# A joint between two runs: weight sums moved to GpSimd, T2's low part by halves, P1 and P6 ahead of the first groups

## The reference

```python
# attention with decay: per head, blocks of 64 tokens, a state carried over
intra = (qb @ kb.T * Dmask) @ vb
inter = (qb * lam_pow) @ kv_state
# mixture: 4 experts, w1[e] 512x1024, w2[e] 1024x512
out += p[:, e:e + 1] * (np.maximum(x @ w1[e], 0.0) @ w2[e])
# projection: two factors, then two matrices
h = (x @ w1) * (x @ w2) @ w3
return h @ w_out
```

## Time and profile before

| what | value |
|---|---|
| median of 3 runs | 796.5 us (796.08 to 797.36) |
| the profiled execution's own time | 793.99 us |
| its span (first to last instruction) | 792.2 us |
| TensorE busy | 776.9 us, 98% |
| VectorE, GpSimd, ScalarE busy | 442.4, 439.7, 207.8 us |
| granted TensorE clock | 1.000 |

### The profile page before, as it was taken

How to read it: one execution, slowest core, us unless ns; L and a number is a source line. 1 busy time by engine, 2 the same in 40 slices (tenths; PEclk the granted TensorE clock), 3 DMA queues, 4 the chain that set the end, 5 groups by cost and what they waited for, 6 DMA issues and landing times.

```text
span 792.2 us, 9983 instructions
## 1 busy us (share of the span) xinstructions
PE 776.9 (98%) x3854; PEld 642.5 (81%) x3854; DVE 442.4 (56%) x627; ACT 207.8 (26%) x292; POOL 439.7 (56%) x389
## 2 busy tenths in 40 slices
PE   9999889999999999999999999999998899999998
PEld 7878768888888888888888888888886788888887
DVE  7549874554545545545545455456378653636356
ACT  7423331122222212221222122122234331223110
POOL 8837586557546565665575565656657533342500
PEclk9999999999999999999999999999999999999999
DMA  9977111010210110210100111101000200100004
GB/s 336 342 260 235 61 73 53 2 53 27 67 53 1 54 55 0 86 40 22 53 23 32 53 41 54 54 0 54 27 26 1 72 11 25 54 28 0 1 1 159
DMA packets 26590, 51.29 MB, mean 65 GB/s; under 512 B 3112, under 2 KB 9008, under 8 KB 26544
## 3 DMA queue, kind: packets, MB, share of 16 engines
q1 hardware_dynamic: 26384, 50.64, 18.9%
q10 hardware_dynamic: 160, 0.02, 0.0%
HBM read 45.38 MB, written 5.28 MB: 64 GB/s over the span
## 4 chain that ended last, share of the span: by engine, by line
PE 92%; DVE 4%; POOL 2%; issue 1%; ACT 0%; ACTq 0%; DVEq 0%
PE banks L1303 41%; PE banks L1276 27%; PE banks L1286 15%; PE banks L1189 5%; PE banks L1201 1%; DVE probs L869 1%; PE banks L1233 1%; PE banks L1225 1%; DVE qs L879 1%; POOL xs_l L524 1%; POOL hl L524 1%; PE banks L1249 0%; DVE t L908 0%; PE banks L1241 0%; POOL w_l L524 0%
## 5 line engine op out<-in xcount | busy, mean ns | idle before, releaser
L1010 DVE TENSOR_TENSOR acc<-banks,acc 128x512 f32<-128x512 f32 x215 | 147.1, 690 | 148.3 <-PE banks L1303 135.8
L524 POOL TENSOR_TENSOR hl<-ring,hh 128x512 fp32r<-128x512 f32 x96 | 138.3, 1454 | 162.1 <-ACT hh L630 162.1
L630 ACT ACTIVATE hh<-ring 128x512 fp32r<-128x512 f32 x120 | 75.7, 632 | 404.6 <-DVE ring L987 345.8
L524 POOL TENSOR_TENSOR w_l<-up_raw,w_h 128x1024 fp32r<-128x1024 f32 x43 | 103.4, 2406 | 90.8 <-ACT w_h L630 90.8
L1303 PE MATMUL banks<-hh,d_h 128*128 128x512 f32 x384 | 149.5, 389 | 2.0 <-POOL hl L524 2.0
L1303 PE MATMUL banks<-hh,d_l 128*128 128x512 f32 x384 | 149.4, 389 | 0.0
L1303 PE MATMUL banks<-hl,d_h 128*128 128x512 f32 x384 | 149.4, 389 | 0.0
L1276 PE MATMUL banks<-xs_h,w_h 128*128 128x512 f32 x336 | 131.2, 390 | 5.5 <-DVE u L968 4.7
L1276 PE MATMUL banks<-xs_h,w_l 128*128 128x512 f32 x336 | 130.8, 389 | 0.0
L1276 PE MATMUL banks<-xs_l,w_h 128*128 128x512 f32 x336 | 130.7, 389 | 0.0
L1303 PEld LDWEIGHTS banks<-hh,d_h 128*128 128x128 f32 x384 | 72.1, 188 | 17.3 <-issue 2.4
(11 more groups left out here) (139 smaller groups left out, 992.7 us busy)
## 6 DMA issues: line engine op xcount, KB each, us to landing
dn_raw<-in_moe_w SPq DMA_DIRECT2D x16, 512.0 KB, 3.3
up_raw<-in_moe_w SPq DMA_DIRECT2D x14, 512.0 KB, 3.3
w_raw<-in_w3T SPq DMA_DIRECT2D x16, 256.0 KB, 6.4
up_raw<-in_w SPq DMA_DIRECT2D x8, 512.0 KB, 3.3
pb<-route_scratch SPq DMA_DIRECT2D x12, 256.0 KB, 3.3
out<-acc SPq DMA_DIRECT2D x11, 256.0 KB, 2.0
wo_raw<-in_w_out SPq DMA_DIRECT2D x8, 256.0 KB, 5.3
chunk_w<-in_kT SPq DMA_DIRECT2D x8, 256.0 KB, 5.3
```

The lines of the kernel that those rows point to most:

```text
L524: return tt(dst, whole, high.bitcast(F32), ALU.subtract)
L630: return nc.scalar.activation(dst, src, ACT.Copy)
L1010: tt(cols, group_bank(g), cols, ALU.add).then_inc(acc_done, 1)
```

## The change

Three things.

At the start, GpSimd makes only the first half of T2's low part; VectorE makes the second half behind `t3_sum(0)`, with a semaphore of its own, `t2_lo`, and the counts of `tp_lo` fall by one. 

For w = 1, TensorE does P1 and P6 first and then groups 0 to 3; VectorE's `sum_u2(1)` goes ahead of the adds of these groups, and GpSimd does `d_low(0)` behind `hidden_low` 2 and not behind `hidden_low` 1.

At the joint, the four sums of run 17's weights go from VectorE to GpSimd, behind `a_low(17)` and ahead of B11's low parts; ScalarE's `s_high(17)` goes from behind the copy of P2 to between the `b_high` of B11 and of B21; VectorE's `weight_sums_low(17)` goes from behind `sum_c22(16)` to between `t4_sum(1)` and `t3_low(1)`.

```diff
--- before.py
+++ after.py
@@ -254,7 +254,8 @@
 
 
         b_hi, b_lo, xc_hi, xc_lo = sem("b_hi"), sem("b_lo"), sem("xc_hi"), sem("xc_lo")
-        t_sum, t_hi, tp_lo, t3_lo = sem("t_sum"), sem("t_hi"), sem("tp_lo"), sem("t3_lo")
+        t_sum, t_hi, tp_lo, t2_lo, t3_lo = (
+            sem("t_sum"), sem("t_hi"), sem("tp_lo"), sem("t2_lo"), sem("t3_lo"))
 
 
         wa_hi, wa_lo, ws_sum, ws_hi, ws_lo = sem("wa_hi"), sem("wa_lo"), sem("ws_sum"), sem("ws_hi"), sem("ws_lo")
@@ -559,7 +560,9 @@
                     low(xs_l[:, which, k, :], src[:, k, :], xs_h[:, which, k, :]).then_inc(tp_lo, 1)
 
             T2_AT, T4_AT = acc[:, 0:KH, 0:CW], acc[:, KH:KT, 0:CW]
-            t_low(0, T2, T2_AT)
+
+            pool.wait_ge(t_hi, 2)
+            low(xs_l[:, T2, 0, :], T2_AT[:, 0, :], xs_h[:, T2, 0, :]).then_inc(tp_lo, 1)
             t_low(0, T4, T4_AT)
 
             def a_low(j):
@@ -601,12 +604,17 @@
                 if later:
                     s_low(w + 1)
                 hidden_low(OUTS * w + 1)
-                d_low(w)
-                for k in range(2, OUTS):
+                if w > 0:
+                    d_low(w)
+                hidden_low(OUTS * w + 2)
+                if w == 0:
+                    d_low(w)
+                for k in range(3, OUTS):
                     hidden_low(OUTS * w + k)
 
 
             a_low(NQ + 1)
+            sums(NQ + 1)
             for which, rows in ((B11, slice(0, KH)), (B21, slice(KH, KT))):
                 for k in range(KH):
                     pool.wait_ge(b_hi, NB + 1 + (which == B21))
@@ -762,6 +770,7 @@
             for d in range(KT):
                 xc_high(d)
             b_high(B11, slice(0, KH), slice(0, CW), grouped(NQ - 1, 0) - KH)
+            s_high(NQ + 1)
             b_high(B21, slice(KH, KT), slice(0, CW), grouped(NQ - 1, 0))
             t_high(1, 0)
 
@@ -784,7 +793,6 @@
                         t_high(1, 3)
                         factor(5, "Ub", bank_u)
                         factor(0, "P2", bank_x)
-                        s_high(w + 1)
                         d_high(hidden_of(w))
                     else:
                         snapshot(w)
@@ -953,6 +961,8 @@
             third_low(NCH - 1)
             t2_sum(0)
             t3_sum(0)
+            dve.wait_ge(t_hi, 2)
+            sub(xs_l[:, T2, 1, :], acc[:, 1, 0:CW], xs_h[:, T2, 1, :]).then_inc(t2_lo, 1)
 
             def sum_u2(w):
                 dve.wait_ge(piece_done, made(w, "P6"))
@@ -1001,9 +1011,10 @@
                 cols = acc[:, d, c * CW:(c + 1) * CW] if Q < NQ else outs[:, ST * c + d, :]
                 if g == 0:
 
-                    dve.wait_ge(tp_lo, 6)
+                    dve.wait_ge(tp_lo, 5)
+                    dve.wait_ge(t2_lo, 1)
                 if g == GR * NQ:
-                    dve.wait_ge(tp_lo, 12)
+                    dve.wait_ge(tp_lo, 11)
                 if Q in (0, NQ):
                     nc.vector.tensor_copy(cols, group_bank(g)).then_inc(acc_done, 1)
                 else:
@@ -1052,8 +1063,11 @@
                     sum_u2(w)
                     gate_piece(2, "Ub", bank_u)
                 else:
-                    add_groups(w - 1, (0, 1, 2, 3))
+                    if w > 1:
+                        add_groups(w - 1, (0, 1, 2, 3))
                     sum_u2(w)
+                    if w == 1:
+                        add_groups(w - 1, (0, 1, 2, 3))
                     add_groups(w - 1, (4, 5))
                     gate_piece(0, "Ua", bank_u)
                     add_groups(w - 1, (6, 7))
@@ -1081,6 +1095,7 @@
             t2_sum(1)
             t3_sum(1)
             t4_sum(1)
+            weight_sums_low(NQ + 1)
             t3_low(1)
 
             def b22_low():
@@ -1103,14 +1118,11 @@
                     sum_u2(w)
                     if w == NQ:
                         b22_low()
-                        weight_sums(w + 1)
                     add_groups(before, (4, 5, 6, 7))
                     sum_u3(w)
 
                     dve.wait_ge(h_lo, n)
                     sum_c22(w, a_tile[3])
-                    if w == NQ:
-                        weight_sums_low(w + 1)
                     sum_c21(w, a_tile[1])
                     sum_c12(w, a_tile[2])
                 else:
@@ -1341,7 +1353,9 @@
                     pe.wait_ge(probs_ready, 2 * NCH)
                 pe.wait_ge(ws_lo, w + 1)
                 if w in (0, NQ):
-                    pe.wait_ge(tp_lo, 4 if w == 0 else 8)
+                    pe.wait_ge(tp_lo, 3 if w == 0 else 7)
+                if w == 0:
+                    pe.wait_ge(t2_lo, 1)
                 product(bank_y, w % 2, S2, T2, True)
 
             def ua(w):
@@ -1380,14 +1394,14 @@
                 else:
                     pe.wait_ge(xc_lo, ST)
                 if w == NQ:
-                    pe.wait_ge(tp_lo, 10)
+                    pe.wait_ge(tp_lo, 9)
                 product(bank_z, w % 2, S1, T1, True)
 
             def p4(w):
 
                 pe.wait_ge(u3_ready, w + 1)
                 if w in (0, NQ):
-                    pe.wait_ge(tp_lo, 6 if w == 0 else 12)
+                    pe.wait_ge(tp_lo, 5 if w == 0 else 11)
                 product(bank_y, w % 2, A22, T4, False)
 
             def p3(w):
@@ -1409,10 +1423,16 @@
             p3(0)
 
             for w in range(1, NQ):
-                groups(w - 1, (0, 1))
-                p1(w)
-                groups(w - 1, (2, 3))
-                p6(w)
+                if w == 1:
+
+                    p1(w)
+                    p6(w)
+                    groups(w - 1, (0, 1, 2, 3))
+                else:
+                    groups(w - 1, (0, 1))
+                    p1(w)
+                    groups(w - 1, (2, 3))
+                    p6(w)
                 groups(w - 1, (4, 5))
                 ua(w)
                 groups(w - 1, (6, 7))
```

## The result

The kernel after takes 791.37 us (median of 4 runs, 791.08 to 791.79) against 796.93 us (4 runs, 796.08 to 798.42): ratio 0.9929, interval 0.9911 to 0.9946. The profiled executions tell another story: span 792.2 before, 789.3 after, 2.9 us apart, as forecast (789.35). So the steps of the sum have to be read first, and then the question is why the medians are 2.7 us further apart than the traces.

The account below looks back on a forecast made before the run. TensorE, busy 98% of the span, was taken as the bound, so only its waits could be gained. Start 2.45 plus joint 0.4 made 2.85 us, taken from the 796.5 median: 793.6, range 791.3 to 795.9.

Parts of the forecast that it names:

- The start: First run, up to the first groups: T2 by halves and P1(1), P6(1) ahead gain 2.45 us, bounds 1.2 and 2.8.
- GpSimd's set: Start: T4 x2, `hl` x2, `d_l` and one more `hl`, needed by the first groups; to end between 112.2 and 113.3.
- up to 0.15 more: Start, P6(0): added to its 0.50 wait because the pipe no longer drains; 0.6 taken.
- this is why moving `d_low` matters: Start: with `d_low` behind `hl` 2 the multiply ends by 109.9, `c21` by 110.6, so P6(1) doesn't wait.
- The joint: Runs 16 and 17: P4(16) at 614.2 instead of 614.60, 0.4 us gained of 3.13; bounds 3.2 gain, 1.0 loss.
- over a microsecond: Joint: P6(16) waits this long for `xs_l` in place of 0.34, at no net cost.
- the slide of B21 onto `t1_sum`: Joint: B21's two subtractions slide from 596 onto `t1_sum` and `t2_sum`, putting VectorE's sums up to 1.2 us later.
- `t4_sum` under T2's first subtraction: Joint: `t4_sum`, made later by B21, falls inside GpSimd's chain and costs up to 1.0 us more.
- bounds of 613.7 - 603.07 = 10.6 and 11.7: Joint: GpSimd's six subtractions from 603.07 with three VectorE operations end at 613.7; `t4_sum` inside adds up to 1.0.
- The sum: Whole kernel: 2.45 + 0.4 = 2.85 us off the profiled execution, span 792.2 to 789.35.
- Rival B: Joint freed: P4(16) starts when P5 is done, 3.2 us gained instead of 0.4, 790.85; chance 0.13.
- its last step: Whole kernel: the profiled execution is 2.5 us below the 796.5 median, from which the same 2.85 is taken: 793.6.

## Why the prediction was wrong, point by point

**The start** was right in mechanism and low by 0.4: 2.83 for 2.45. P6(0) did not wait, the first group did not wait at all (0.0 to 0.4 forecast), P1(1) and P6(1) ran directly behind P3(0). On the old axis the first group came at 112.96 - 0.11 = 112.85, for 113.1. Two terms were mis-sized. 0.1 of it is GpSimd's set: I let it end between 112.2 and 113.3, it ended at 112.12, since VectorE's new instruction got the port first and was through in 0.69. The larger part is TensorE's own. I took 110.86, where the last recorded duration ends, for the moment at which it was free; but that matmul began at 110.48, and with a spacing of 0.23 the next can begin at 110.71. So the recorded idle time of 1.97 cost 2.12, and the first matmul behind it took 0.31 to the next instead of 0.23: that wait cost 0.23 more than its idle time. I had added this for P6(0) ("up to 0.15 more") and left it out for the first group. The step "this is why moving `d_low` matters" fell: in the old place `c21` is 1 us later and P6(1) waits a few hundredths. Nothing was late behind it; groups 4 to 11 don't wait.

**The joint** was right: 0.30 us (0.15 in the trace with the lower clock) for 0.4, in place of a wait of 3.13. P6(16)'s new wait is 1.97 ("over a microsecond"), P4(16) is released by GpSimd's `xs_l` where the clock stays full (in the other trace the slower matmuls reach past T4's low part, and it shows no wait), P4(17) still waits 1.53. The sums, the slide of B21 onto `t1_sum`, `t4_sum` under T2's first subtraction and `weight_sums_low` stretched to 2.32 are all in the trace. GpSimd's chain, from T2's first subtraction to T4's last, took 611.49 - 600.36 = 11.1 us, for bounds of 613.7 - 603.07 = 10.6 and 11.7.

**The sum** gave the span to 0.1 us (789.35, measured 789.3). So close a hit is in part luck: the start gave 0.4 more, the joint 0.25 less, and P1(0) came 0.11 late.

**Rival B** had the number, 790.85, and not the reason: its 3.2 us at the joint are 0.15 to 0.30 in the traces, and at full clock P4(16) was held by T4's low part as forecast.

**What failed** is its last step, "that execution is 2.5 us below the median of the runs, from which I take the same". The 2.5 us were no constant around the kernel. They are a second form of the kernel before: 52 of 76 executions lay in the upper group, each with a granted clock below 1.000, and the execution of this kind that was profiled lost 2.84 us to TensorE's lower clock behind the 3.13 us wait at P4(16). The trace shown was of the other form, with a clock of 1.00 from end to end, so no row of it showed the loss, though its own time, below every one of the three runs beside it, was the sign that something was missing from it. With the change that wait and the loss are gone: 2.9 us from the waits and some 2.7 from the clock are the 5.6 measured. Either half of the change alone takes away most of the loss. A wait priced only by its length was the error; no rival had a clock in it. The Trainium skill (TensorE: Matmul & The Clock Gate, Part 1) says that the gate drops TensorE to half rate when it idles, and that the number of slow matmuls at a kernel's start differs from run to run of one kernel. The traces agree, deep in the kernel: 14 and none in two executions of the kernel before, behind the same wait. With that I should have held a rival of 796.5 - 2.85 - 2.5 = 791.2, for which the only evidence was the 2.5 us.

**Open** is what decides, in one execution, whether the lower clock comes and for how many matmuls. That the wait's place in time has a part in it is likely from the two kernels that moved it without changing it (2 of 8 and 11 of 12 executions with a lower clock, against 52 of 76), but it is not shown, and the rule was not looked for. Open too is the last microsecond of spread at a clock of 1.000 with all waits filled.

## What to carry to other kernels

A profiled execution that is faster than all timed ones may be one of two forms of the kernel: look at the granted clock of the timed executions, and at a trace of the other form, before pricing a wait. Here a wait of 3.1 us on TensorE cost 2.8 more in clock in the middle of the executions in which it fell, and one of 2 us some 1.4 to 1.5. Such a loss is free where another wait follows it, and dear where the chain runs through it. When an engine in a shared-port chain is relieved, write down what moves up: the next operation took the place of the one removed, twice.

## What the hardware showed that was not expected

A wait of 3.13 us was followed by 14 matmuls 0.43 us apart instead of 0.23 (6 us long, 2.84 lost). It was followed by about 8 (1.60 and 1.63 lost) in one execution each of two kernels in which it came 2.7 and 0.7 us earlier, counted from P1(0), and by none in a third of the executions of the kernel before. Waits of 1.97 us at P6(16) brought it in three of five traces in which they were not filled. In the 76 executions of the kernel before, the medians of the two groups lie 2.8 us apart (794.0 and 796.8), with no overlap in granted clock.

Between VectorE and GpSimd, a VectorE operation of 1024 columns cost GpSimd's chain some 0.9 us (11.1 against 10.2 with `weight_sums_low` out of it) and not its 1.22, while the one of the two that waited had its wait inside its recorded duration: 0.73 -> 1.30, 1.22 -> 3.11.
